# Raw weights land where their lower parts will stand, the first block means come from a matmul, and the feed-forward follows four attention steps

## The reference

```python
# attention, B=2, H=8, S=768, D=64; block=32, window=16
k_sum = k.reshape(B, H, nb, block, D).max(axis=3)
v_sum = v.reshape(B, H, nb, block, D).mean(axis=3)
scores_l = scale * q @ k^T, kept where |i - j| < window
scores_s = scale * q @ k_sum^T + log(block)
a = softmax([scores_l, scores_s]);  x = a @ [v, v_sum]
# feed-forward on 1536 tokens x 512
h = max(x @ w1, x @ w2, x @ w3)          # 768 wide
x = h @ w_out
# experts: skip score, gate over 8 experts, top one
out = x + gate * (relu(x @ w1[e]) @ w2[e])   where x @ w_skip > 0
```

## Time and profile before

| | us |
|---|---|
| median of 3 runs | 536.09 |
| profiled execution, own time | 535.93 |
| its span, first to last instruction | 534.1 |
| first feed-forward matmul starts | 42.24 |
| step 10 starts (group 0 done, group 1 next) | 99.87 |
| group 5's first matmul starts | 274.01 |
| last feed-forward matmul ends | 312.18 |
| TensorE busy | 465.2 (87%) |
| VectorE, ScalarE, GpSimd busy | 209.0, 179.6, 79.9 |

### The profile page before, as it was taken

The page is one execution under the profiler, slowest core; times in us unless marked ns, Lnnn a source line. Parts: engine busy times, 40 slices in busy tenths (PEclk is TensorE's granted clock), DMA queues, the critical chain, the costliest instruction groups (busy, mean ns, idle before and its releaser), DMA issues.

```text
span 534.1 us, 9695 instructions
## 1 busy us (share of the span) xinstructions
PE 465.2 (87%) x3409; PEld 401.6 (75%) x3410; DVE 209.0 (39%) x475; ACT 179.6 (34%) x461; POOL 79.9 (15%) x99
## 2 busy tenths in 40 slices
PE   1557868999999999999999951698999999999974
PEld 1337867899899899999999941476777777787753
DVE  5674457343333323412302237627422222222371
ACT  2585333443433243333111113427222222222360
POOL 2641003322010000010000000011111111111111
PEclk9988879999999999999999975799999999999998
DMA  8747431242130112020020024944611111111000
GB/s 262 254 135 243 139 110 56 56 135 76 29 105 26 39 45 97 16 80 1 14 80 1 2 79 178 360 152 147 216 50 39 39 39 39 39 39 35 22 15 2
DMA packets 20239, 46.64 MB, mean 87 GB/s; under 512 B 3580, under 2 KB 7164, under 8 KB 20208
## 3 DMA queue, kind: packets, MB, share of 16 engines
q1 hardware_dynamic: 16944, 35.25, 19.5%
q0 software_dynamic: 2400, 6.24, 3.5%
q10 hardware_dynamic: 864, 4.72, 2.6%
HBM read 37.86 MB, written 9.96 MB: 90 GB/s over the span
## 4 chain that ended last, share of the span: by engine, by line
PE 77%; DVE 6%; DMA 5%; issue 5%; ACT 3%; SPq 1%; DVEq 1%; POOL 1%; ACTq 0%; POOLq 0%
PE bank L497 29%; PE pair L613 14%; PE bank L603 12%; PE bank L512 9%; PE bank L446 2%; PE pair L416 2%; PE bank L595 2%; PE bank L434 2%; PE bank L539 2%; DMA raw_w<-ffn_w_dram 2%; DMA k_all<-k_all_dram 1%; DMA rows<-x_rows,index_next 1%; DMA e_raw<-experts_dram 1%; DVE e_lo L918 1%; ACT w_hi L668 1%
## 5 line engine op out<-in xcount | busy, mean ns | idle before, releaser
L497 PE MATMUL bank<-x_hi,w_hi 128*128 128x256 f32 x432 | 129.1, 299 | 10.1 <-DVE h_m L860 10.1
L497 PE MATMUL bank<-x_lo,w_hi 128*128 128x256 f32 x432 | 124.4, 288 | 0.0
L497 PE MATMUL bank<-x_hi,w_lo 128*128 128x256 f32 x432 | 124.3, 288 | 0.0
L497 PEld LDWEIGHTS bank<-x_hi,w_hi 128*128 128x128 f32 x432 | 85.0, 197 | 13.4 <-DVE h_m L860 10.5
L497 PEld LDWEIGHTS bank<-x_lo,w_hi 128*128 128x128 f32 x432 | 85.0, 197 | 0.1
L497 PEld LDWEIGHTS bank<-x_hi,w_lo 128*128 128x128 f32 x432 | 84.8, 196 | 0.0
L1142 POOL DMA_INDIRECT rows<-x_rows,index_next x16 | 16.5, 1032 | 244.7 <-DVE index_next L1067 155.9
L613 PE MATMUL pair<-e_hi,u_hi 128*128 128x512 f32 x112 | 48.3, 431 | 4.5 <-DVE u_lo L1064 3.5
L1064 DVE TENSOR_TENSOR u_lo<-bank,u_hi 128x512 fp32r<-128x512 f32 x28 | 19.3, 691 | 82.1 <-ACT u_hi L747 82.1
L603 PE MATMUL bank<-e_hi,r_hi 128*128 128x512 f32 x112 | 46.5, 415 | 3.7 <-DVE e_lo L918 2.1
L1108 POOL TENSOR_TENSOR probs<-probs,rowinv 128x480 f32<-128x480 f32 x24 | 25.6, 1067 | 160.2 <-DVE rowinv L817 160.2
(11 more groups left out here) (153 smaller groups left out, 750.4 us busy)
## 6 DMA issues: line engine op xcount, KB each, us to landing
e_raw<-experts_dram SPq DMA_DIRECT2D x24, 512.0 KB, 5.6
v_w<-v_dram SPq DMA_DIRECT2D x24, 192.0 KB, 2.5
raw_w<-ffn_w_dram ACTq DMA_DIRECT2D x6, 768.0 KB, 4.4
k_all<-k_all_dram SPq DMA_DIRECT2D x8, 400.0 KB, 4.3
q_t<-q_dram SPq DMA_DIRECT2D x24, 128.0 KB, 3.0
v_all<-v_all_dram SPq DMA_DIRECT2D x8, 384.0 KB, 6.2
x_rows<-y_rows SPq DMA_DIRECT2D x12, 256.0 KB, 2.3
out_dram<-y_rows SPq DMA_DIRECT2D x12, 256.0 KB, 2.3
```

Of the source, the lines that this page charges most:

```text
L497: mm = pe.matmul(ring_of(gr, n)[:, 0:GT], w_parts[a][:, f, (w * KD + k) * P:(w * KD + k + 1) * P], x_parts[c][:, gr % XS, k, :], start=i = ...
```

## The change

Six edits go together:

1. `raw_w` goes. `w_raw` is a tensor at the very addresses of `w_lo`, with all eight pieces: each piece lands where its lower part will stand, and the subtraction writes over its own input. No landing waits for a split any more. All eight loads are in SyncE's list. Piece 0 is loaded and split in three parts, one for each of w1, w2, w3.
2. ScalarE rounds piece f+1 after the first unit of slice f (`weights_high`), the two pieces of w_out after units 15 and 17. VectorE subtracts pieces 1, 2, 4, 6, 7. GpSimd subtracts pieces 3 and 5 (`W_POOL`).
3. The block means of the first batch come from six matmuls of 512 columns (`sum_values`): 128 tokens of `v_nat` by the columns of a selecting matrix `v_sel` with 1/32 in it, accumulated in one bank, and placed by ScalarE (`place_means`). The second batch keeps the way before, in steps 8 to 12.
4. Group 0 of the feed-forward begins in step 4 instead of 6. Scores run one step ahead instead of two; `values(g)` stands in step g instead of g+1. The fourth step of a cycle has its first part empty.
5. `place_keys` moves from VectorE to GpSimd and is done for each step (4 tiles of 96 keys and 24 maxima) instead of for each pair (12 tiles).
6. The first steps are written out by hand on each engine, the mask is loaded in two halves, `q_t` has six slots instead of four, `k_all` four buffers instead of two.

The core of the diff:

```diff
-        PARTS = (cut(0, 2, 4, 6), cut(6, 8, 10, 12), cut(12, 14, 16, 18), cut(18, 19, 19, 20))
+        PARTS = (cut(0, 2, 4, 6), cut(6, 8, 10, 12), cut(12, 14, 16, 18), cut(18, 18, 19, 20))
-        FIRST = PPB + LEAD
+        FIRST = PPB
+        W_POOL = (3, 5)
-        raw_w = place("raw_w", [P, RAW, WCH])
+        at["w_raw"] = at["top"]
         w_lo = place("w_lo", [P, WPIECES, WCH], F32R)
+        w_raw = place("w_raw", [P, WPIECES, WCH], F32, "w_raw")
...
 (TensorE)
+            def sum_values(j):
+                if j % 2 == 0:
+                    pe.wait_ge(v_nat_in[j // 2], 16)
+                first = (VT - 1 - j) * QUAD
+                mm = pe.matmul(ps_sums, v_sel[:, first:first + KC], v_nat[:, j, :], start=j == 0, stop=j == VT - 1)
...
             def step(g):
-                if g + 2 < STEPS:
-                    scores(g + 2)
+                if g + 1 < STEPS:
+                    scores(g + 1)
                 for n in parts[0]:
                     unit(gr, n)
                 turn_probs(g)
                 for n in parts[1]:
                     unit(gr, n)
-                if g > 0:
-                    values(g - 1)
+                values(g)
                 for n in parts[2]:
                     unit(gr, n)
...
             def up_unit(gr, n):
-                if n % 3 == 0 and gr == 0:
-                    pe.wait_ge(w_lo_done, f + 1)
+                if gr == 0 and f == 0:
+                    pe.wait_ge(w_lo_done, n + 1)
+                if gr == 0 and n % 3 == 0:
+                    weights_split(f)
...
 (ScalarE)
             def weights_high(i):
-                act.wait_ge(raw_w_in[i % RAW], 16 * (i // RAW + 1))
-                act.copy(w_hi[:, i, :], raw_w[:, i % RAW, :]).then_inc(w_hi_done, 1)
-                if 2 <= i + 1 < WPIECES:
-                    load_raw(act, i + 1)
+                act.wait_ge(raw_w_in[i], 16)
+                act.copy(w_hi[:, i, :], raw_of(i)).then_inc(w_hi_done, 1)
...
             def step(g):
                 if g in SUM_TURN:
                     place_sums(SUM_TURN[g])
-                if g > 1:
-                    x_high(g - 2)
+                for n in parts[0]:
+                    unit(gr, n)
                 if g + 1 < STEPS:
                     exps(g + 1)
-                for n in parts[0]:
-                    unit(gr, n)
+                turned_probs(g)
                 for n in parts[1]:
                     unit(gr, n)
+                x_high(g)
                 for n in parts[2]:
                     unit(gr, n)
...
                     act.copy(h_a[:], ring_of(gr, n)[:, 0:GT]).then_inc(h_a_done, 1)
+                    if gr == 0 and f + 1 < KF:
+                        weights_high(f + 1)
                     if f >= 1:
                         hidden_hi(gr, f - 1)
+                if gr == 0 and n in (UPS - 3, UPS - 1):
+                    weights_high(KF + (n == UPS - 1))
...
 (VectorE)
             def step(g):
+                if g + 1 < STEPS:
+                    mask_max(g + 1)
+                for n in parts[0]:
+                    unit(gr, n)
                 if g in KEY_MAX:
                     key_max(KEY_MAX[g])
-                    place_keys(KEY_MAX[g])
-                if g + 2 < STEPS:
-                    mask_max(g + 2)
-                if g > 1:
-                    x_low(g - 2)
+                for n in parts[1]:
+                    unit(gr, n)
                 if g + 1 < STEPS:
                     invert(g + 1)
+                x_low(g)
...
 (GpSimd)
+            def weights_low(i):
+                pool.wait_ge(w_hi_done, 3 + i)
+                pool.tensor_tensor(w_lo[:, i, :], raw_of(i), w_hi[:, i, :].bitcast(F32), ALU.subtract
+                                   ).then_inc(w_lo_done_pool, 1)
...
+            for g in range(FIRST, STEPS):
+                if g + 2 < STEPS:
+                    place_keys(g + 2)
+                if g == PPB:
+                    weights_low(W_POOL[0])
+                if g in VALUE_SUMS:
+                    value_sums(VALUE_SUMS[g])
                 if g + 1 < STEPS:
                     norm(g + 1)
+                if g == PPB + 1:
+                    weights_low(W_POOL[1])
```

More of the change, by code:

```diff
@@ L316, in ring_of, with third, by_vector, raw_of @@
             return ps_ring[(UNITS * gr + n) % len(ps_ring)]
-        def load_raw(eng, piece):
-            at_least(eng, w_lo_done, piece - RAW + 1)
-            eng.dma_start(raw_w[:, piece % RAW, :], dram["ffn_w"][piece]).then_inc(raw_w_in[piece % RAW], 16)
+        def third(t):
+            return slice(t * THIRD, (t + 1) * THIRD)
+        def by_vector(i):
+            return 3 + sum(j not in W_POOL for j in range(1, i + 1))
+        def raw_of(i):
+            return w_raw[:, i, :]
         @block.sync
@@ L385, in _ @@
+            for s in range(PPB, STEPS):
+                if s + PPB < STEPS:
+                    load_queries(s + PPB)
+                    load_values(s + PPB)
+                if s in (4, 5, 8, 9):
+                    load_all_values({4: 4, 5: 5, 8: 6, 9: 7}[s])
+                if 6 <= s < 6 + PPB:
+                    load_all_keys(s - 6 + PPB)
+                if s >= 8 and s % PPB == 0:
+                    store_rows((s - 8) // PPB)
             sp.wait_ge(x_lo_done, GQ)
@@ L388, in _ @@
                 sp.dma_start(t[:], dram[name]).then_inc(route_consts_in, 16)
-            for gr in range((STEPS - 10) // PPB + 1, GROUPS):
+            for gr in range((STEPS - 8) // PPB, GROUPS):
                 store_rows(gr)
@@ L544, in _ @@
             scores(1)
+            scores(2)
+            sum_values(0)
+            sum_values(1)
             pe.wait_ge(ident_in, 16)
-            for g in range(STEPS):
+            turn_probs(0)
+            scores(3)
+            sum_values(2)
+            sum_values(3)
+            turn_probs(1)
+            sum_values(4)
+            sum_values(5)
+            values(0)
+            turn_probs(2)
+            values(1)
+            scores(4)
+            turn_probs(3)
+            values(2)
+            values(3)
+            for g in range(FIRST, STEPS):
                 step(g)
-            values(STEPS - 1)
-            for n in range(PARTS[PPB - LEAD][0][0], UNITS):
-                unit(GROUPS - 2, n)
             gr = GROUPS - 1
@@ L881, in _ @@
             key_max(0)
-            place_keys(0)
+            dve.wait_ge(mask_in[0], 16)
+            mask_max(0)
             key_max(1)
-            place_keys(1)
-            dve.wait_ge(consts_in, 16)
-            mask_max(0)
+            key_max(2)
             mask_max(1)
             invert(0)
-            for g in range(STEPS):
+            key_max(3)
+            mask_max(2)
+            invert(1)
+            mask_max(3)
+            invert(2)
+            invert(3)
+            x_low(0)
+            x_low(1)
+            first_weights_low(0)
+            dve.wait_ge(mask_in[1], 16)
+            mask_max(4)
+            x_low(2)
+            first_weights_low(1)
+            x_low(3)
+            first_weights_low(2)
+            invert(4)
+            for g in range(FIRST, STEPS):
                 step(g)
-            for n in range(PARTS[PPB - LEAD][0][0], UNITS):
-                unit(GROUPS - 2, n)
             for n in range(UNITS):
```

260 lines of the change are left out of this document (161 added, 99 removed).

## The result

The changed kernel takes 528.77 us (median of 4 runs, 528.09 to 530.59) against 535.93 (534.63 to 537.84) for the kernel before on the same chip: ratio 0.9869, 95% interval 0.983 to 0.9908. That is faster, by 7.2 us, and 2.8 us above the forecast of 526. The profiled execution took 528.9, its span is 527.1.

What follows compares the result with a forecast made beforehand. TensorE was taken to bound the kernel from step 10 on, with the loss ahead of 99.87 us. Terms -11.7 - 4.0 + 3.8 + 1.6 = -10.3 from 535.93 gave 525.6, forecast as 526; range 519 to 532.

Steps and rivals of the forecast that it cites:

- Term A: Start, up to the feed-forward's first matmul: 42.2 to 30.5 us, set by the compute chain, not loading; gain 11.7.
- Term B: Feed-forward group 0: 57.6 to 53.6 us, 42.0 without stalls plus 11.6 of stalls, mostly behind weight pieces; gain 4.0.
- Term C: Behind group 0: 16 attention steps stand there, two more than before; loss 3.8 us.
- Term D: Down units of groups 1 to 4: ScalarE's exponentials and copy precede the last h_hi; loss 0.4 each, 1.6 us.
- Rival 1: Group 0: GpSimd's piece costs little, so step 5's product isn't late; 519 us, chance 0.14.
- Rival 2: Start hardly moves, through slow sums, late small transfers or ScalarE's list: start at 36, 531.5 us, chance 0.15.
- Rival 3: Every step: the shorter lead makes TensorE wait before each turn, 1.0 us over 20 steps; 546 us, chance 0.06.
- Rival 4: Group 0: VectorE and GpSimd lock each other out, making it 3.5 us longer; 529.5 us, chance 0.10.

Runs made afterwards that it cites:

- r2: The changed kernel unchanged, executed once more for a second profile: 529.72 us.
- e4: The changed kernel with four of the six `sum_values` matmuls left out: 513.04 us, with a whole expert block missing, so total time isn't comparable.
- e1: The changed kernel with GpSimd's product for step 5 put ahead of its subtraction of weight piece 3: 524.96 us, ratio 0.9787 to the kernel before.
- e2: The changed kernel with weight pieces 3 and 5 subtracted by VectorE, none by GpSimd: 521.54 us, ratio 0.9712 to the kernel before.
- e5: The changed kernel with ScalarE rounding the last hidden slice ahead of the exponentials in every group but the last: 524.82 us, ratio 0.9756 to the kernel before.
- e6: The changed kernel with the edits of e2 and e5 together, and pieces 6 and 7 taken earlier: 513.78 us, ratio 0.957 to the kernel before.

## Why the prediction was right, and where it was off

**Term A, the start to 30.5: right in size and in its holder, though the chain ran 1.4 late.** It came out at 30.52 (30.13 in r2). The sums and the values behind them, in TensorE's order after:

```profile
12.38 3.77 PE L475 MATMUL bank<-v_nat,v_sel 128*120 128x512 f32 x4
...
17.83 1.98 PE L475 MATMUL bank<-v_nat,v_sel 128*120 128x512 f32 x4
...
20.09 1.88 PE L475 MATMUL bank<-v_nat,v_sel 128*120 128x512 f32 x4
23.04 0.69 PE L504 MATMUL bank<-probs_t,v_w 120*64 120x64 f32 x16 [1.08 <-ACT v_w L747]
```

ScalarE's list at the same place: the copy of turn 1, the end of step 3's exponentials, the placing of the means:

```profile
20.29 0.58 ACT L762 COPY probs_t<-bank 120x512 f32<-120x512 f32 x1 [1.14 <-PE bank L492]
...
22.20 0.19 ACT L726 ACTIVATION_READ_ACCUMULATOR probs<-probs,negmax 128x1 f32 x1
22.41 1.06 ACT L747 COPY v_w<-bank 24x512 f32<-24x512 f32 x2
```

The last sums end at 21.97, but ScalarE isn't free before 22.39 and goes straight on to the placing: it, not the sums, releases values 0, as predicted, at 23.04 instead of 21.6. It is late because its copy of turn 1 waited for TensorE, and turn 1 stands behind four of the sums. The prediction had that too; its marks against the measured ones show where the 1.4 came in: first sums start at 12.2 and 12.38, turn 0 at 15.2 and 15.95, second sums at 16.4 and 17.83, turn 1 at 18.2 and 19.65. So the first pair took 1.8 for each matmul where the sum has 1.5 (it says nearly twice 0.85, which would be up to 1.7), and turn 0 and scores 3 took 1.88 together where it has 1.2. Both ran at nearly twice the time that the same work takes a little later (second pair 0.91 from start to start, as taken; a turn 0.44), so I read it as half clock, though the granted clock is given as 1.00 for that stretch. From values 0 on the chain had the predicted spacing: values 1, 2 and 3 at 24.75, 26.53 and 28.91 against 23.3, 25.2 and 27.4. They are 1.3 to 1.5 late throughout, which is just what was allowed for "handoffs" and GpSimd's copies; the number held by luck in this, because an allowance covered slow matmuls. e4 fits this chain: with no sums ahead of it turn 1 started at 15.92, ScalarE was free at 19.2, and there it waited for the two sums that were left.

**Term B, group 0 to 53.6: mechanism right, size off by 2.3.** The stalls, predicted and measured: piece 3, 4.7 and 4.90; piece 5, 1.6 (its own terms, 5.2 less 3.5, give 1.7) and 2.13; step 7's turn, 1.2 and 1.1; first down unit, 2.5 and 2.4; in all 10.0 and 10.7 with 0.2 elsewhere. GpSimd's piece took 3.42 and 3.46, taken as 3.3 from two slopes of the earlier trace rows. The mis-sized term is the half clock behind the long wait: 1.6 for 24 matmuls, where the turn ahead of them is slow too and the matmuls took 4.85: 2.5. The remaining 0.7 is in neither (restarts behind waits, by elimination; not tested). In r2 the same group took 58.15, so the size also holds for one execution only. e1 and e2 confirm the mechanism: the product moved ahead takes away the wait of 4.9 and the half clock behind it, no GpSimd piece takes away both waits.

**Term C, two more steps, 3.8: right.** Group 4, which now holds the steps that the shorter lead pushes in, took 43.83 instead of 39.90, 3.9.

**Term D, 0.4 in each down unit.** Three waits of 1.5 us in all in groups 1 to 3 and none in group 4 (the rows above): groups 1 to 3 took 136.6 instead of 134.2, 2.4 for the 1.2 predicted, of which 1.7 is waits and the rest longer matmul time, put down to the restarts. The clause was right, its size half of what it is. e5 shows that the order alone makes it: there groups 1 to 3 took 134.3. It takes away the 2.4 of group 0 too, but most of that went into the new wait of 1.0 and a first stretch at half clock (0.55 from 29.5 to 33 us); the FFN end comes 3.8 earlier, 1.0 of it from an earlier start.

The sum by marks is then -11.7 - 1.7 + 3.9 + 2.4 = -7.1 against -10.3.

**The rivals.** Rival 1 (GpSimd's piece costs little): no, 3.42. Rival 2 (the start hardly moves): no, though its sums were slower than taken. Rival 3 (a wait in each step): no; the steady stretch has 43.43 busy of 44.00, and the missing 0.57 is the down unit's. Rival 4, the lock: its price of 529.5 is nearer to the measured 528.8 than the forecast is, but not for its reason: GpSimd's pieces started straight behind ScalarE's roundings and took 3.42 and 3.46. Where it shows most, it cost nothing. VectorE's h_lo ran beside GpSimd's piece 5:

```profile
65.33 1.91 DVE L968 TENSOR_TENSOR h_lo<-h_m,h_hi 128x256 fp32r<-128x256 f32 x1
```

1.91 for an operation of 0.42: held until GpSimd's piece of 63.50 ended near 67.0. Its result wasn't yet wanted. The Trainium skill (SBUF — State Buffer, "Who interferes with whom") says that whichever of the two issues first keeps the other out until it has finished; the trace agrees, here with GpSimd first and VectorE kept out. It did cost a little elsewhere: VectorE's piece 7, begun at 73.49 while GpSimd had a product from 73.02 to 74.01, took 2.12 instead of 1.76 and is in the chain that ends the down unit's wait of 2.4, up to 0.4 us.

**What stays open.** Why the same first transfers land at 7.02 to 9.29 us; no experiment touched it. Whether e6's half clock at the feed-forward's start (first matmul 0.58, at 29.15) can be kept away. What before's wait for pieces is in the mean: it was 10.1 us in one profile and 12.4 in the other, so the row on which term B's old side rests is itself uncertain by some 2 us.

## What to carry to other kernels

Before a piece of work is handed to a slower, idle engine, look at what stands behind it in that engine's list: GpSimd idled for 11 us and still made TensorE wait 4.9, because the piece came ahead of a product that TensorE wanted; the engine that had lost the work had room for it. When a stall goes, list what each engine has to do before the next due time: here four new waits of 1 to 5 us together equalled the three removed, and moving a few lines in an engine's list took most of them away (1.8 us are left in e6). A number that comes out right can rest on an allowance that hides an error; compare the intermediate marks too.

## What the hardware showed that was not expected

The first transfers of an execution vary: keys 1, with the same instructions ahead, were in use between 7.02 and 9.29 us in six profiles, and the kernel before carries nearly all of it into its start. For the changed kernel that isn't shown either way: in its two profiles and in those of e1, e2, e5 and e6 GpSimd's copy took keys 1 at 7.00 to 7.76, and the starts, 29.1 to 30.5, don't follow them; none of them had a landing as late as 9.29.

The clock doesn't repeat from execution to execution, and a wait can come and go with it. In r2 the waits of 4.9, 2.1 and 2.4 us are as in after to within 0.1. But the same wait of 2.13 us for piece 5 stands at 67.02, and 1.2 us behind its end TensorE fell to half clock, while in the first profile of the same kernel it stayed at 1.00. From 67 (r2: 67.2) to 72 us, first in after, then in r2:

```profile
67.00:72.00 5.00, 4.99 (x51) 4.79 (x52) 1.35 (x2) 3.20 (x5) 0.81 (x2) 1.00 0.31 116
```

```profile
67.20:72.00 4.80, 4.80 (x38) 4.46 (x39) 0.86 (x2) 2.89 (x5) 0.62 (x2) 0.64 0.20 53
```

38 matmuls instead of 51 in about the same width. Most of that was given back at once: after waited 1.1 us for step 7's product, r2 came later and didn't wait, and its down unit began only 0.3 behind (74.77 against 74.47). What r2 lost stands behind the down unit's wait of 2.4: there the same 41 matmuls took 7.40 us at a granted clock of 0.77 instead of 5.86 at 1.00. So r2's group 0 took 2.2 us longer, and its feed-forward ended at 306.9 although it started 0.4 earlier. Slow matmuls ahead of a wait for another engine can thus be free, and behind the last such wait they count in full.

In e1 the wait for piece 5, 2.13 us again, had half clock behind it from the first matmul. So one wait of this length was followed by full clock, by half clock after 1.2 us and by half clock at once in three profiles. The spread of the runs fits a price by chance, without proving it: e2 and e6, without the waits for GpSimd's pieces, lie within 1.5 and 1.7 us from lowest to highest, e1 and e5, with them, within 6.0 and 4.4; but after itself, with them too, lies within 2.5 in its four runs.
